# Scores ahead of the turn in tile 0's attention, w_out rounded one pair later, w_in's splits shared by VectorE and GpSimd, bounds loaded on two queues

## What is computed

```python
scores = scale * np.matmul(q, k.transpose(0, 1, 3, 2))
keep = is_global | is_local          # 8 global keys, 96 local ones
scores = np.where(keep, scores + bias, -1e9); a = softmax(scores)
x = np.matmul(a, v)                  # (1536, 512) once the heads stand side by side

h = x @ w_in                         # 512 -> 1024
solu = h * softmax(h)
y = layer_norm(solu) * g_ln @ w_out  # 1024 -> 512

yn = y / rms(y) * rms_g
out = (silu(yn @ w_gate) * (yn @ w_val)) @ w_down   # 512 -> 1536 -> 512
```

## Time and profile before

| | |
|---|---|
| median of three runs | 596.2 us |
| the profiled execution: its own time | 596.7 us |
| its span, first to last instruction | 594.9 us |
| busy: TensorE, VectorE, ScalarE, GpSimd | 568.3, 302.5, 257.9, 83.6 us |
| mean granted clock of TensorE | 0.990 |

### The profile page before, as it was taken

The page is one execution under the profiler, slowest core; times in us unless marked ns, Lnnn a source line. Parts: engine busy times, 40 slices in busy tenths (PEclk is TensorE's granted clock), DMA queues, the critical chain, the costliest instruction groups (busy, mean ns, idle before and its releaser), DMA issues.

```text
span 594.9 us, 10707 instructions
## 1 busy us (share of the span) xinstructions
PE 568.3 (96%) x3697; PEld 512.5 (86%) x3697; DVE 302.5 (51%) x778; ACT 257.9 (43%) x598; POOL 83.6 (14%) x223
## 2 busy tenths in 40 slices
PE   2887999999999999999999999999999999999997
PEld 1876888888888888878899999999999999999996
DVE  4757878777877798767455223222222222221211
ACT  3646766665666677645454212222221222222112
POOL 4440221222212204213010010001001000100000
PEclk9998899999999999999999999999999999999999
DMA  8656554532443243333431100020020000000000
GB/s 215 191 146 179 148 158 119 149 101 73 124 135 108 80 126 100 99 115 108 174 109 72 64 9 2 1 71 1 1 71 0 0 0 35 0 0 36 2 1 35
DMA packets 21613, 46.95 MB, mean 79 GB/s; under 512 B 2764, under 2 KB 2776, under 8 KB 21576
## 3 DMA queue, kind: packets, MB, share of 16 engines
q1 hardware_dynamic: 21264, 46.47, 26.2%
q10 hardware_dynamic: 312, 0.01, 0.0%
HBM read 40.18 MB, written 6.29 MB: 78 GB/s over the span
## 4 chain that ended last, share of the span: by engine, by line
PE 78%; DVE 11%; issue 4%; POOL 3%; ACT 2%; DMA 2%; ACTq 0%; DVEq 0%; SPq 0%
PE hidden L410 9%; PE hidden L411 8%; PE hidden L412 8%; PE mixed L1246 5%; PE mixed L410 3%; PE mixed L411 3%; PE scores_b L410 3%; PE scores_b L411 3%; PE scores_b L412 3%; PE mixed L412 3%; PE turned L410 3%; PE turned L411 3%; PE scores_a L410 3%; PE scores_a L411 3%; PE turned L412 3%
## 5 line engine op out<-in xcount | busy, mean ns | idle before, releaser
L731 ACT ACTIVATE act_hi<-act_sb 128x256 fp32r<-128x256 f32 x72 | 30.1, 418 | 108.8 <-DVE act_sb L1104 108.8
L1104 DVE TENSOR_TENSOR act_sb<-mixed,silu 128x256 f32<-128x256 f32 x36 | 15.3, 425 | 93.7 <-PE mixed L412 93.1
L1246 PEld LDWEIGHTS mixed<-v_in,probs_t 116*128 116x128 f32 x384 | 55.1, 210 | 8.3 <-ACT probs_t L682 4.5
L1104 DVE TENSOR_TENSOR act_sb<-turned,silu 128x256 f32<-128x256 f32 x36 | 15.3, 424 | 89.3 <-PE turned L412 86.8
L1246 PE MATMUL mixed<-v_in,probs_t 116*128 116x64 f32 x384 | 54.1, 289 | 3.4 <-ACT probs_t L682 3.4
L410 PE MATMUL hidden<-down_hi,act_hi 128*128 128x512 f32 x144 | 57.0, 396 | 0.3 <-DVE act_lo L1109 0.2
L411 PE MATMUL hidden<-down_lo,act_hi 128*128 128x512 f32 x144 | 56.9, 395 | 0.0
L412 PE MATMUL hidden<-down_hi,act_lo 128*128 128x512 f32 x144 | 56.7, 394 | 0.0
L682 ACT ACTIVATE probs_t<-turned 116x512 f32<-116x512 f32 x48 | 28.6, 596 | 63.6 <-PE turned L1231 63.6
L672 ACT ACTIVATE probs<-logits,neg_max 128x232 f32<-128x232 f32 x96 | 45.7, 481 | 6.6 <-DVE neg_max L995 6.6
L1109 DVE TENSOR_TENSOR act_lo<-act_sb,act_hi 128x256 fp32r<-128x256 f32 x72 | 30.6, 425 | 34.9 <-ACT act_hi L731 34.9
(11 more groups left out here) (145 smaller groups left out, 1544.3 us busy)
## 6 DMA issues: line engine op xcount, KB each, us to landing
qk_raw<-qk_pairs SPq DMA_DIRECT2D x96, 180.0 KB, 3.2
v_in<-v_windows SPq DMA_DIRECT2D x12, 448.0 KB
staging<-w_gate SPq DMA_DIRECT2D x3, 1024.0 KB, 6.4
staging<-w_val SPq DMA_DIRECT2D x3, 1024.0 KB, 5.6
y_spill<-y_out SPq DMA_DIRECT2D x12, 256.0 KB, 4.3
staging<-w_down SPq DMA_DIRECT2D x3, 1024.0 KB, 6.0
y_in<-y_spill SPq DMA_DIRECT2D x6, 512.0 KB, 3.7
out<-o_sb SPq DMA_DIRECT2D x12, 256.0 KB, 2.1
```

The costliest lines, as they stand in the source:

```text
L731: nc.scalar.activation(act_hi[:, slot], act_sb[:, slot], ACT.Copy).then_inc(act_rounded, 1)
L1104: nc.vector.tensor_tensor(act_sb[:, slot], val_ps[slot][:, 0:WIDE], silu[:, slot], ALU.mult).then_inc(act_ready, 1)
L1246: ins = pe.matmul(mixed[:, head * d:(head + 1) * d], probs_t[:, p % 2, h, half], v_in[:, even, half, head * d:(head + 1) * d], start=(half ...
```

## The change

1. In `one_tile(-1)` TensorE makes the scores of pair n + 1 ahead of the turn of pair n, where it made them between the turn and the mix.
2. ScalarE rounds the four halves of w_out (blocks 2 and 3) one pair slot later, and VectorE's splits of them, which follow one slot behind, move with them. The last one, of block 3, now stands at slot (1, 3), the end of tile 1.
3. Each w_in block is split half by VectorE and half by GpSimd, with a semaphore for each block. VectorE's half of block 1 stands at slot (0, 1); its second half of block 0, at slot (0, 0), is gone. GpSimd does its half of block 0 in the middle of the eight bias products, and the logits of tile 1 wait for two, four, six and eight of these instead of all eight at once.
4. n_local is loaded by SP, ahead of everything, and n_global by ScalarE as before. The three small operations that find out whether the general case applies come first on VectorE; each engine reads the result earlier (ScalarE ahead of its first exponential).
5. SP loads block 1 ahead of the last two q/k loads of `one_tile(-1)`, not behind them.

```diff
@@ PE, one_tile, t < 0
+                        score_pair(n + 1, (p + 1) % pairs)
                         turn_pair(n, p)
-                        score_pair(n + 1, (p + 1) % pairs)
                         mix_pair(a, 1 - even, p)
@@ the tables of halves
         round_1 = {(-1, 1): [(0, 0)], (-1, 2): [(0, 1)], (0, 0): [(1, 0), (1, 1)],
-                   (0, 2): [(2, 0)], (0, 3): [(2, 1)], (1, 0): [(3, 0)], (1, 1): [(3, 1)],
+                   (0, 3): [(2, 0)], (1, 0): [(2, 1)], (1, 1): [(3, 0)], (1, 2): [(3, 1)],
...
         split_1 = {divmod(pairs * t + p + 1, pairs): halves for (t, p), halves in round_1.items()}
-        del split_1[0, 1]
+        del split_1[-1, 3]
+        split_1[0, 1] = [(1, 0)]
@@ SP
+            sp.dma_start(bounds_i[:, 1, :], n_local.bitcast(I32).partition_broadcast(P)).then_inc(bounds_in, 16)
             for p in range(pairs):
                 load_qk(0, p)
...
+                if known(t) and t < 0:
+                    load_block(sp, 1)
                 for p in range(pairs):
...
-                if known(t) and t < 0:
-                    load_block(sp, 1)
@@ GpSimd
+            def split_half(c):
+
+                hi, lo, raw, _ = half_block(c, 1)
+                pool.wait_ge(w_rounded, 2 * c + 2)
+                pool.tensor_tensor(lo, raw, hi.bitcast(F32), ALU.subtract).then_inc(w_in_split[c], 1)
...
-            for half in range(2):
-                hi, lo, raw, _ = half_block(1, half)
-                pool.wait_ge(w_rounded, 2 * 1 + half + 1)
-                pool.tensor_tensor(lo, raw, hi.bitcast(F32), ALU.subtract).then_inc(w_in1_split, 1)
+                if h == heads // 2 - 1:
+                    split_half(0)
+            split_half(1)
@@ ScalarE
-            exp_pair(0, 0, 0)
             act.wait_ge(general_known, 1)
...
+            exp_pair(0, 0, 0)
             for t in range(-AHEAD, LOOP_FROM):
@@ VectorE
-                if known(n) and n == pairs:
-                    dve.wait_ge(bias_others, heads)
+                if known(n) and pairs <= n < 2 * pairs:
+                    dve.wait_ge(bias_others, 2 * (p + 1))
...
+            find_general()
             start_distance(0)
             split_qk(0, 0)
             finish_distance(0)
             set_bias()
             take_logits(0, 0, 0)
-            find_general()
             split_qk(1, 1)
```

More of the change, by code:

```diff
@@ L213, in fused_kernel @@
         w_split = sem("w_split")
-        w_in1_split = sem("w_in1_split")
+        w_in_split = [sem("w_in0_split"), sem("w_in1_split")]
         qk_loaded = [sem(f"qk_loaded_{p}") for p in range(pairs)]
@@ L335, in wait_split @@
         def wait_split(engine, c):
-            if c == 1:
-                engine.wait_ge(w_in1_split, 2)
+            if c < N1:
+                engine.wait_ge(w_in_split[c], 2)
             else:
-                engine.wait_ge(w_split, 2 if c == 0 else 2 * c)
+                engine.wait_ge(w_split, 2 * (c - N1 + 1))
         def load_block(sp, c):
@@ L385, in split_block @@
             if gain is None:
-                nc.vector.tensor_tensor(lo, raw, hi, ALU.subtract).then_inc(w_split, 1)
+                nc.vector.tensor_tensor(lo, raw, hi, ALU.subtract
+                                        ).then_inc(w_in_split[c] if c < N1 else w_split, 1)
                 return
@@ L786, in one_step @@
                         round_block(act, c, half)
-            for i, n in enumerate((n_global, n_local)):
-                act.dma_start(bounds_i[:, i, :], n.bitcast(I32).partition_broadcast(P)).then_inc(bounds_in, 16)
+            act.dma_start(bounds_i[:, 0, :], n_global.bitcast(I32).partition_broadcast(P)).then_inc(bounds_in, 16)
             act.dma_start(gain_rows[0:K1], g_ln.rearrange("(k p) -> k p", p=P)).then_inc(gains_loaded, 16)
@@ L844, in _, with find_general @@
                                            in1=bounds_f[:, :, 0], op0=ALU.mult, op1=ALU.add).then_inc(setup, 1)
+            def find_general():
+                dve.wait_ge(setup, 3)
+                nc.vector.tensor_scalar(general_f[:], bounds[:, 0:1], float(GLOBAL), None, ALU.is_gt).then_inc(setup, 1)
+                dve.wait_ge(setup, 4)
+                nc.vector.scalar_tensor_tensor(out=general_f[:], in0=bounds[:, 1:2], scalar=float(PREV + 1),
+                                               in1=general_f[:], op0=ALU.is_gt, op1=ALU.max).then_inc(setup, 1)
+                dve.wait_ge(setup, 5)
+                nc.vector.scalar_tensor_tensor(out=general_i[:], in0=bounds[:, 1:2], scalar=1.0,
+                                               in1=general_f[:], op0=ALU.is_lt, op1=ALU.max).then_inc(general_known, 1)
             DIST_STEPS = 7
-            DISTANCE = (3, 12)
             def start_distance(v):
-                at = DISTANCE[v]
+                at = 5 + DIST_STEPS * v
                 dve.wait_ge(iota_done, 7)
@@ L881, in set_bias @@
                                             ).then_inc(bias_first, 1)
[L883 to L886, removed]
-                nc.vector.scalar_tensor_tensor(out=general_f[:], in0=bounds[:, 1:2], scalar=float(PREV + 1),
-                                               in1=general_f[:], op0=ALU.is_gt, op1=ALU.max).then_inc(setup, 1)
-                dve.wait_ge(setup, 12)
-                nc.vector.scalar_tensor_tensor(out=general_i[:], in0=bounds[:, 1:2], scalar=1.0,
-                                               in1=general_f[:], op0=ALU.is_lt, op1=ALU.max).then_inc(general_known, 1)
             def general_attention():
```

## The result

| | before | changed |
|---|---|---|
| median of four executions each | 595.59 us | 602.86 us |
| all of them | 594.82 to 596.42 | 600.8, 601.8, 603.91, 604.75 |
| the profiled execution: its own time, span | 596.7, 594.9 | 600.8, 599.0 |
| mean granted clock | 0.990 | 0.986 |

The ratio is 1.0121, 95% interval [1.0080, 1.0162]: slower by 7.2 us. The four executions of the changed kernel lie 4 us apart, and the profiled one is the fastest of them; its span is 4.1 us above that of before. So the two profiles explain 4.1 us. These two are differences between executions of one kernel, which the two profiles can't explain.

A forecast was written before the change was run, and what follows sets the result against it. TensorE was taken to bound the kernel, far ahead of VectorE. Terms 0.5 + 0.8 - 1.8 + 3.1 = +2.6, with +1.5 for the clock +4.1 on 596.2: 600.3 us, wide range 596.8 to 603.2, the forecast's own 599 to 602.5.

The forecast's parts named there:

- Tile 0's attention: Tile 0's pairs: new order makes a pair 4.59 us with 1.04 idle, turn of x at 32.1 against 31.58: +0.5 us.
- w_in's split: w_in's second block: VectorE's half, held up by GpSimd's bias copy, ends at 44.3 where TensorE wants it at 43.50: +0.8 us.
- The tail: Tile 0's tail: w_out's rounding and split leave the way, so tile 1's turn of x comes earlier: -1.8 us.
- The start of tile 2: Tile 2's turn of x: w_out's last split delays VectorE (1.3) and SP's queue (1.8): +3.1 us.
- The clock: Behind the wait at tile 2's start: the granted clock falls, costing +1.5 us (0 to 3.1).
- No fall: Rival, tile 2's start: the stall comes without a clock fall, +2.6, 598.8 us; chance 0.22.
- The fall in tile 0's tail goes: Rival, tile 0's tail: clock falls there no more, 2.2 us comes back, +0.4, 596.6 us; chance 0.10.
- A late first rise: Rival, at the wait for w_in: clock's first rise comes later, 1.6 us on top, 601.9 us; chance 0.12.

The follow-up runs named there:

- x_wval: Changed kernel, but SP issues w_val's load at the head of tile 8's turn instead of the end of tile 1's: 597.39 us, ratio 1.0042 to before.
- b_wout: Kernel before with only the roundings and splits of w_out's four halves one pair slot later: 601.49 us, ratio 1.0083.
- b_wout_wval: Kernel before with w_out's four halves one pair slot later and w_val's load issued at the head of tile 8: 596.05 us, ratio 1.0004.
- b_scores: Kernel before with only the scores ahead of the turn in tile 0's attention: 595.56 us, ratio 1.0000.
- x_scores: Changed kernel with tile 0's attention in the old order (turn, next scores, mix): 601.83 us, ratio 1.0102 to before.
- b_start: Kernel before with only n_local loaded by SP first, the general case found first, and w_in's second load earlier: 593.78 us, ratio 0.9978.
- x_all: Changed kernel with w_val's load late (tile 8), w_in shared as before and tile 0's attention in the old order: 595.33 us, ratio 0.9990 to before.
- best: Kernel before with bounds and general case early, and only the first half of w_out one slot later: 592.6 us, ratio 0.9950.
- b_win: Kernel before with only each w_in block split half by VectorE and half by GpSimd: 597.11 us, ratio 1.0034.
- x_win: Changed kernel with w_in's splits shared as before (VectorE block 0, GpSimd block 1): 601.18 us, ratio 1.0103 to before.
- x_wout: Changed kernel with w_out's roundings and splits in the pair slots of the kernel before: 600.49 us, ratio 1.0075 to before.
- x_fill: Changed kernel with 32 more transposes of the identity on TensorE behind tile 1's last mix: 601.3 us, ratio 1.0088 to before.

## Why the prediction was right

The forecast was 600.3, and the median is 602.9: within the wide range (596.8 to 603.2), but above the 599 to 602.5 that the forecast gave itself, and +7.2 us where +4.1 was forecast. The mechanism was right: a split moved into VectorE's way to tile 2's x, SP's queue held up by the same split, and a fall of the clock behind the wait (with the queue and without it: the changed kernel and x_wval, b_wout and b_wout_wval). The size was too small, in what the clock costs: 1.5 for the fall at tile 2, and nothing for w_in, whose effect was set against the tail's. By the prediction's own steps, in the profile:

- *Tile 0's attention, +0.5*: +0.15 (31.73). A pair takes 4.45 and not 4.59. The idle before a mix, 0.69, is no gain against the forecast 1.04: the trace counts it from the end of the turn, which is 0.35 behind its last issue. From the start of the turn to the mix it is 1.74 (forecast 1.79), and scores and mix are a little shorter than forecast too. The size of this part hides two larger ones: alone, the new order costs 0.82 (b_scores), or 1.65 when the other parts are there (x_scores), and bounds and w_in's half bring 0.64 to 1.06 and 0.70 (b_start, x_all and best; b_win). That VectorE's w_in half gone from ahead of x gives nothing was right only as long as the new order is in. (The half that is gone stood at pair slot (-1, 3); the text on the change says (0, 0).)
- *w_in's split, +0.8*: 44.36 against 43.50 makes +0.86, but the +0.15 of tile 0 is in it, so the term itself is +0.71. The forecast end of 44.3 was a place, too, and the sum added the +0.5 of tile 0 to it once more: the two terms together were put at +1.3 and came to +0.86. The chain came out by its steps: GpSimd's copy ran from 40.38 to 42.12, k_lo began at 40.82 and took 1.79, and VectorE's half ended at 43.08 + 1.23 = 44.31, as forecast. The Trainium skill (SBUF — State Buffer, "Who interferes with whom") says that a VectorE instruction with two SBUF inputs and a GpSimd instruction that reads SBUF exclude one another; the trace agrees, with 1.79 against the 0.64 that k_lo takes elsewhere. What I had not seen is that the price depends on the clock. In some profiles the clock has risen by 40 us (the product at 39.97 takes 0.40), and TensorE is there at 42: then the wait is 2.39, and taking it back brings tile 1's turn 2.36 forward (x_win). In others it rises with the wait (x_wval, x_wout, x_fill, b_win) and the wait is 0.3 to 0.6. This first rise is read from how long a product takes; the granted clock of the table doesn't show it (from 38 to 44 us it reads 1.00 in the profile of before, where the products take 0.63).
- *The tail, -1.8*: from 44.36 to 57.07 it is 12.71, from 43.50 to 58.30 it was 14.80: -2.1, the edge of what was given. The mix waits 1.17 and not 2.39.
- *The start of tile 2, +3.1*: +3.85 from one turn of x to the next. The sum of the four terms was +2.6, and tile 2's turn is 2.62 later. That these agree so well is luck: the terms measured +0.15, +0.71, -2.09 and +3.85, and three that came out lower than forecast make up for the fourth. Of the 3.92 of wait VectorE's part is the 1.48 that x_wval leaves (forecast 1.3), and the queue's the other 2.4 (1.8). SP's signal was forecast for 82.9 as if nothing ahead had moved; it came at 82.4. The work ahead was 1.2 earlier, and so w_val's wait ended 1.05 earlier than forecast (78.62 against 79.67); the issues behind it took 3.8 and not 3.2.
- *The clock, +1.5*: right in kind and too small. By the mark, the four profiles with a wait of 3.92 at tile 2 fell behind it and lost 1.8, 2.7, 3.65 and 3.8; the ones with 1.48 or less lost nothing, and neither did x_fill. The mean of the four is 3.0. With it the forecast would have been 601.8. I had read the price of a fall from one execution, and halved it because the queue was denser. In four profiles, each of another kernel, it lay between 1.8 and 3.8; the profiled execution of the changed kernel, the fastest of its four, shows the smallest. That it varies as much between executions of one kernel is argued from this and not shown.
- *The rivals.* "No fall" is excluded by x_fill and x_wval: without the fall, 601.3 and 597.4. "The fall in tile 0's tail goes" didn't happen in any of the fourteen profiles, with the mix's wait at 1.17 or at 2.4. Where the mix waits less, the clock fell at that mix all the same (the changed kernel, where its eight matmuls take 1.92 and not 1.10, and x_scores), or TensorE then waited 1.9 for x and it fell behind that (the seven others). "A late first rise" was half right: the wait at w_in can disturb the clock, but by another fall (x_scores), not by a later rise; in the changed kernel's profile the rise was earlier than before. So it was wrong to let two clock effects cancel without a price for either.

What stays open: alone, the parts make +4.9, +2.0, 0.0 (or +0.8, by the groups of b_scores) and -1.3, in all +5.6 to +6.4, where the whole makes +7.2 (4.8 to 9.7 by its interval). And x_wout, which has all but w_out's slots, is +4.5 where its parts make +0.7 to +1.5. In x_wout's profile it is +0.7 at tile 1's turn and +1.7 at tile 2's, since the slow stretch between them lasts longer (granted clock 0.83 from 66 to 70 us, before 1.00). The rest is in other executions, and their mean granted clocks say more. Of the kernels without a wait of 3.9 at tile 2, those with w_in's splits as before never had one below 0.990 (123 executions). Those with the splits shared had a second group of times, 2.4 to 3.1 us higher and at a lower clock: b_win in four of twelve executions (0.982 to 0.985), x_wval in four of twelve (0.986 to 0.989), x_fill in three of six (0.986), x_wout in four of six (0.982 to 0.985). So sharing w_in's splits brings a further loss in a third to two thirds of the executions, by itself and not only together with the other parts. A further fall of the clock behind the wait for VectorE's half, as in x_scores' profile, would be such a loss; no execution of these upper groups has a profile, so that this is the place isn't shown.

## What to carry to other kernels

Before a step is moved, list what is issued behind each of its waiters, on every queue: here a split moved by one slot cost VectorE 1.5 us, and SP's queue, whose load waited for it, 2.4 more; moving only the half that stood in the way, with the bounds early, made the kernel 3 us faster (best; 1.3 of that by the bounds). Price a new wait of some 4 us in a dense stretch with its own length and a further loss for the clock behind it, 1.8 to 3.8 us in the four profiles here. And where the executions of a kernel spread more than before (4.0 us in four here, 2.7 in 69 then), one profile shows only one of the outcomes: look at the single times and their mean granted clocks too.

## What the runs showed of the hardware

- The same wait had different prices in four kernels. 3.92, 3.92, 3.93 and 3.93 us of wait at one place in the program lost 1.8, 3.8, 3.65 and 2.7 us in the slow stretch behind (the changed kernel, b_wout, x_win, x_scores).
- Waits of 1.47 to 1.48 at that place lost nothing (three kernels), while a wait of 1.9 for tile 1's x, with one of 1.2 ahead of it, was followed by a slow stretch in every kernel that had it.
- Where the clock rises first isn't fixed: with near the same work ahead of it, the second group of w_in's products took 0.40 each in seven of the fourteen profiles and 0.63 in the other seven. Where the rise is early and w_in's splits are as before, TensorE takes up w_in's second block 1.7 earlier with tile 0's turn of x in the same place (b_wout 41.83, b_wout_wval 41.77, before 43.50).
- The times of one kernel fall into groups and don't spread evenly: before lay at 594.4 to 595.2 or 596.0 to 597.1 us, x_wval at 596.6 to 597.7 or 599.4 to 599.6, b_win at 596.3 to 597.4 or 599.6 to 600.0. There are two kinds. The groups of before are 1.7 apart and have the same mean granted clock (0.990 to 0.991). They go with the first rise: of the eight kernels with w_in's splits as before, the profiled execution of the five with the early rise lies among the lower times of its kernel (b_start, x_all, b_wout_wval, x_win; that of b_wout is 1.5 below its two highest), and that of the three with the late one among the higher ones (before, b_scores, best). The groups of x_wval and b_win are 2.4 and 3.1 apart, and their upper ones have a lower mean granted clock. Both are found by comparing; neither cause was tested.
